# Linear attention ahead of a routed and a dense feed-forward stage: the attention's units put into another order, with smaller tensor tiles for states and turning back

## The reference, cut to what matters

```python
def _attn_ref(q, k, v, alpha):                 # each (4, 8, 768, 48), float32
    state = np.zeros((B, H, D, D)); y = np.zeros_like(q)
    for t in range(S):
        state = alpha[:, :, t, :, None] * state + np.einsum('bhd,bhe->bhde', k[:, :, t], v[:, :, t])
        y[:, :, t] = np.einsum('bhd,bhde->bhe', q[:, :, t], state)
    return y

def reference(...):
    attn_out = _attn_ref(**attn_kwargs)
    x = attn_out.transpose(0, 2, 1, 3).reshape(B * S, H * D)     # 3072 tokens x 384
    x = _moe_ref(x=x, **moe_kwargs)       # normalise, logits against 8 expert vectors, best expert, its relu MLP
    return _moe2_ref(x=x, **moe2_kwargs)  # max of three products with 768 columns, then a product back
```

## Time and profile before

| | us |
|---|---|
| median of 3 runs | 787.59 |
| the runs | 788.26, 786.61, 787.59 |
| the profiled execution | 788.2 |
| its span in the trace | 786.4 |
| end of the attention (last `xc` copied) | 185.86 |

### The profile page before, as it was taken

How to read it: one execution, slowest core, us unless ns; L and a number is a source line. 1 busy time by engine, 2 the same in 40 slices (tenths; PEclk the granted TensorE clock), 3 DMA queues, 4 the chain that set the end, 5 groups by cost and what they waited for, 6 DMA issues and landing times.

```text
span 786.4 us, 15500 instructions
## 1 busy us (share of the span) xinstructions
PE 740.0 (94%) x4774; PEld 652.3 (83%) x4775; DVE 379.5 (48%) x708; ACT 272.5 (35%) x638; POOL 295.8 (38%) x226
## 2 busy tenths in 40 slices
PE   4999999994699999999999999999999999999995
PEld 3888888883499999999999887888888888888885
DVE  6788888865853343333334229433333233333321
ACT  6778888865222222222222231211111112112110
POOL 3243444300382755736358489113133131220011
PEclk9999999997799999999999999999999999999998
DMA  9967675504393443516050220101101010000001
GB/s 181 266 138 180 119 169 106 148 2 144 122 345 128 162 158 133 194 47 218 22 210 31 83 63 21 31 11 40 31 31 51 10 40 30 20 20 0 11 21 50
DMA packets 128790, 74.49 MB, mean 95 GB/s; under 512 B 103448, under 2 KB 122016, under 8 KB 128736
## 3 DMA queue, kind: packets, MB, share of 16 engines
q1 hardware_dynamic: 118624, 53.53, 25.2%
q0 software_dynamic: 4096, 10.24, 3.5%
q10 hardware_dynamic: 6016, 10.07, 3.5%
HBM read 59.03 MB, written 14.79 MB: 94 GB/s over the span
## 4 chain that ended last, share of the span: by engine, by line
PE 77%; issue 13%; DVE 5%; POOL 2%; ACT 1%; DMA 0%; DVEq 0%; POOLq 0%; ACTq 0%
PE bank L1424 54%; PE bank L1223 4%; PE bank L1253 3%; PE bank L1460 3%; PE bank L1316 3%; PE bank L1305 3%; PE bank L1284 2%; PE bank L1297 2%; DVE Sm L893 1%; PE bank L1271 1%; PE bank L1410 1%; POOL out L529 1%; PE bank L1482 1%; DVE A L863 1%; DVE low1h L1044 1%
## 5 line engine op out<-in xcount | busy, mean ns | idle before, releaser
L489 POOL TENSOR_TENSOR wsp<-raw,wsp 128x1536 f32 x28 | 103.8, 3727 | 91.6 <-DVE wsp L1109 91.6
L1424 PE MATMUL bank<-yh,mh 128*128 128x512 f32 x324 | 128.2, 396 | 0.1
L1424 PE MATMUL bank<-yh,ml 128*128 128x512 f32 x324 | 126.5, 390 | 0.0
L529 POOL DMA_INDIRECT out<-oo,tok_t x24 | 24.3, 1011 | 202.5 <-DVE oo L1166 202.5
L1424 PE MATMUL bank<-yl,mh 128*128 128x512 f32 x324 | 91.4, 390 | 0.0
L1424 PE MATMUL bank<-wsp,xh 128*128 (+1 forms) x324 | 85.3, 398 | 3.7 <-issue 3.2
L1424 PE MATMUL bank<-wsp,hTh 128*128 x432 | 81.8, 340 | 0.0
L811 ACT CAST gh<-t 128x512 fp32r<-128x512 f32 x36 | 22.3, 620 | 155.3 <-DVE t L1177 155.3
L1424 PEld LDWEIGHTS bank<-wsp,hTh 128*128 128x128 f32 x432 | 73.9, 188 | 0.2 <-issue 0.2
L1424 PEld LDWEIGHTS bank<-wsp,xh 128*128 128x128 f32 x324 | 58.9, 188 | 15.9 <-issue 4.1
L1424 PEld LDWEIGHTS bank<-yl,mh 128*128 128x128 f32 x324 | 60.8, 188 | 12.9
(11 more groups left out here) (207 smaller groups left out, 1315.4 us busy)
## 6 DMA issues: line engine op xcount, KB each, us to landing
raw<-in_moe_w SPq DMA_DIRECT2D x16, 1536.0 KB, 8.0
expert_rows<-ye ACTq DMA_DIRECT2D x27, 193.0 KB
yg<-expert_rows SPq DMA_DIRECT2D x24, 193.0 KB
nat<-in_alpha SPq DMA_DIRECT2D x32, 144.0 KB, 2.9
nat<-in_k SPq DMA_DIRECT2D x32, 144.0 KB, 3.0
nat<-in_q SPq DMA_DIRECT2D x32, 144.0 KB, 3.0
vt<-in_v SPq DMA_DIRECT2D x32, 144.0 KB, 3.1
attention_rows<-xc SPq DMA_DIRECT2D x4, 1152.0 KB, 5.5
```

The costliest lines, as they stand in the source:

```text
L489: g.tensor_tensor(wsp[:, ds(to, 1), 1, n, part], raw[:, n:n + 1, part], wsp[:, ds(to, 1), 0, n, part].bitcast(f32), ALU.subtract).then_inc ...
L529: g.indirect_dma_start(out=out, out_offset=bass.IndirectOffsetOnAxis(ap=tok_t[:, i, 0:1], axis=0), in_=oo[i % 2][:], in_offset=None).then_ ...
L1424: last = mm(o, x, y, start=(n == 0), stop=(n == len(todo) - 1))
```

## The change

PE's order within a unit becomes: turn `kp`, all scores together, states, results, turn the results of unit u-1 back, carries, turn alpha of u+4, turn q of u+1, turn k of u+2.

- The scores of a unit go to four banks of PSUM (chunks 0 to 3 to banks 6 and 7, chunks 4 and 5 to banks 0 and 1), and DVE masks them with three instructions of 512 elements over two banks each, where it had four of 384.
- States are made per head in tiles of 64 columns: ten products of 48 columns in place of five of 96. `UA` and `V` become 48 wide.
- Turning back is done in four quadrants of 64 by 64: 24 products with N = 56 in place of six with N = 104. It takes the results of the unit before, and those of the last unit are turned back behind the loop. The logits come in eight parts to a token instead of four, so that the reductions at L949 read twice as much. `stage_x` and `store_x` run one unit later.
- DVE's order within a unit becomes three masks, states, scans of u+3, q of u+1, inverse and k of u+2.
- Alpha of unit u+4 is turned (and so needed) at the end of unit u; it was u+3. Alpha, k and q of u+4 are loaded once q of u is turned, v once the results of u are made.
- The first loads stand in the order in which they are needed; two small loads and one alpha are issued by ACT. The norm of the expert vectors is taken with squares on DVE and Ln and Exp on ACT, pads of two buffer sets are written by POOL, and the loops over batches are written out.
- The flag's product moves from the middle of the last unit to its very start.

The core of the diff; `step` is DVE's, and from `back` on it is PE's:

```diff
+        for u in range(NU - UPB):
+            j = u % UPB
+            sp.wait_ge(pe_q, 2 * u + 2)
+            for n in range(3):
+                load_one(u + UPB, j, n)
+            sp.wait_ge(pe_Y, CR + 2 * u + 2)
+            load_one(u + UPB, j, 3)
+            if u and j == 0:
+                store_x(u // UPB - 1)
...
+        def step(u):
+            j = u % UPB
+            for part in range(3):
+                mask(u, j, part)
+            states(u, j)
+            if u + 3 < NU:
+                scans(u + 3, (j + 3) % UPB)
+            if u + 1 < NU:
+                scale_q(u + 1, (j + 1) % UPB)
+            if u + 2 < NU:
+                recip(u + 2, (j + 2) % UPB)
+                scale_k(u + 2, (j + 2) % UPB)
...
+        def back(y, j, b0, c):
+            for half in range(2):
+                rows = slice(HL * half, HL * half + HL)
+                for hd in range(2):
+                    sl = slice(HL * hd, HL * hd + HL)
+                    yield mm(bank[b0 + hd][rows, (D + E) * c:(D + E) * c + D + E], y[sl, c, rows], read[sl, j, :],
+                             start=True, stop=True)
...
             for c in range(CH - 1):
-                last = mm(bank[4 + c // 4][:, HD * (c % 4):HD * (c % 4) + HD].rearrange("p (h d) -> p h d", h=2),
-                          kpT[:, c, :], vt[j][:, c, :, 0:D], start=True, stop=True)
+                for hd in range(2):
+                    rows = slice(HL * hd, HL * hd + HL)
+                    last = mm(bank[4][rows, D * c:D * c + D], kpT[:, c, rows], vt[j][:, c, hd, 0:D],
+                              start=True, stop=True)
             last.then_inc(pe_U, 1)
-            scores(u, j, 1)
...
+            if u:
+                turn_back(u - 1, (j - 1) % UPB)
             for cc in range(1, CH):
...
+            if u + 4 < NU:
+                turn_alpha(u + 4, j, 4)
+            if u + 1 < NU:
+                turn_q(u + 1, (j + 1) % UPB)
+            if u + 2 < NU:
+                turn_k(u + 2, (j + 2) % UPB)
```

More of the change, by code:

```diff
@@ L75, in build @@
     embp = sb("embp", [E, H * HL])
-    read = sb("read", [P, UPB, HD + E])
+    read = sb("read", [P, UPB, D + E])
     es = sb("es", [E, 8])
@@ L217, in build @@
     assert max(attention_end, router_end, experts_end) <= router_const
-    bank = [nc.alloc_psum_tensor(f"bank{i}", [P, 512], f32) for i in range(8)]
+    pair = [nc.alloc_psum_tensor(f"bank{2 * i}_{2 * i + 1}", [P, 2, 512], f32) for i in range(4)]
+    bank = [pair[i // 2][:, i % 2, :] for i in range(8)]
     sem = {}
@@ L329, in _ @@
                          ).then_inc(w0_in, 16)
[L330 to L335, removed]
+        for u in range(NU - UPB):
[7 more added lines that the diff above has]
+                store_x(u // UPB - 1)
+        store_x(B - 2)
         store_x(B - 1)
@@ L429, in _ @@
         pool.sem_inc(const_ready, 1)
+        for j in range(2, NAT):
+            g.memset(nat[j][:, 0, :, :, D:HL], 1.0)
+            g.memset(nat[j][:, 1:3, :, :, D:HL], 0.0)
+            g.memset(vt[j][:, :, :, D:HL], 0.0).then_inc(late_pads, 1)
         def decay(u, j):
@@ L847, in _ @@
             d.memset(vt[j][:, :, :, D:HL], 0.0).then_inc(pads_ready, 1)
+        dve.wait_ge(emb_in, 16)
+        link(d.tensor_tensor(sq[0:E, :], embn[:], embn[:], ALU.mult))
+        d.tensor_reduce(es[:, 0:1], sq[0:E, :], AX.X, ALU.add).then_inc(e_sq, 1)
+        link(d.memset(embp[:], 0.0))
+        dve.wait_ge(ident_ready, 1)
+        for jj in range(UPB):
+            d.tensor_tensor(read[:, jj, 0:D], ident[:, 0:D], ident[:, HL:HL + D], ALU.add)
         dve.wait_ge(e_act, 1)
@@ L1214, in _, with keep_warm @@
         mm, tr = nc.tensor.matmul, nc.tensor.transpose
+        def keep_warm(n, to):
+            for _ in range(n):
+                mm(to[:, 0:HC * P], before[:], causal[:].rearrange("p c n -> p (c n)"), start=True, stop=True)
         pe.wait_ge(ident_ready, 1)
-        pe.wait_ge(pads_ready, NAT)
+        pe.wait_ge(pads_ready, 2)
         def turn(u, j, n, h, dst, done):
@@ L1272, in unit, with scores @@
                 last.then_inc(pe_kT, 1)
+        def scores(u, j):
             pe.wait_ge(dve_qp, CR + 2 * u + 2)
-            pe.wait_ge(act_X, CR + 2 * u)
-            scores(u, j, 0)
-            pe.wait_ge(act_kT, CR + 2 * u + 2)
-            if flag:
+            pe.wait_ge(act_X, CR + 2 * (u - 2) + 2)
+            r = [slice(0, D), slice(HL, HL + D)]
+            for c in range(CH):
+                to = pair[3][:, :, P * c:P * c + P] if c < 4 else pair[0][:, :, P * (c - 4):P * (c - 4) + P]
+                cc = slice(P * c, P * c + P)
+                for hd in range(2):
+                    last = mm(to[:, hd, :], kp[j % 2][r[hd], cc], qp[j % 2][r[hd], cc], start=True, stop=True)
+                    if c in (3, CH - 1):
+                        last.then_inc(pe_S, 1)
@@ L1300, in unit @@
+            for cc in range(CH):
+                if cc % 2 == 0:
+                    pe.wait_ge(dve_S, CR + 3 * u + cc // 2 + 1)
+                for hd in range(2):
+                    mm(out(cc)[HL * hd:HL * hd + HL], vt[j][:, cc, hd, :], Sm[j % 2][:, hd, cc, :],
+                       start=(cc % HC == 0), stop=(cc == 0), skip_group_check=True)
+            if u:
+                turn_back(u - 1, (j - 1) % UPB)
             for cc in range(1, CH):
                 pe.wait_ge(act_UA, CR + 5 * u + cc)
-                pe.sem_inc(pe_carry, 1)
@@ L1380, in _ @@
                     pe.wait_ge(s_yTc, u + 1)
+                    pe.sem_inc(pe_carry, 1)
                     for c in range(CH):
-                        o = (HD + E) * (c % HC)
-                        last = mm(bank[2 + c // HC][:, o:o + HD + E], yT[0][:, c, :], read[:, j, :], start=True, stop=True)
+                        for last in back(yT[0], j, 2, c):
+                            pass
                     last.then_inc(s_X, 1)
@@ L1397, in _ @@
         last.then_inc(r_ss, 1)
-        def keep_warm(n):
-            for _ in range(n):
-                mm(bank[3][:, 0:HC * P], before[:], causal[:].rearrange("p c n -> p (c n)"), start=True, stop=True)
         def lift_x(slot, need, par):
```

288 lines of the change are left out of this document (130 added, 158 removed).

## The result

The changed kernel is faster, by less than half of what was forecast: 781.58 us (median of 8 runs, 777.36 to 784.60) against 786.48 for the kernel before (8 runs, 784.81 to 788.26). The ratio is 0.9931, 95% interval 0.9904 to 0.9958. When it was run a second time, beside the first experiments, it took 779.08 (6 runs) and 0.9912 (0.9890 to 0.9934). Its runs lie 7.2 us apart, those of before 3.5. The profiled execution took 779.84, its span is 778.1 where that of before was 786.4.

A forecast was written before the change was run, and what follows sets the result against it. PE was taken to bound the attention, busy 10.05 of 10.35 us a unit. Units, start, restart, stores, end and last reduction gave 788.2 - 20.7 + 5.4 + 2.4 + 1.0 - 2.5 + 0.4 = 774.2, own range 769 to 779.

The forecast's parts named there:

- -14.0: Whole kernel: the forecast terms' sum in us against the profiled execution of the kernel before, 788.2 to 774.2.
- the end: From unit 12's start to the last copy: 36.5 us instead of 39.0, -2.5, with a 3.6 us wait for the flag.
- the stores: Batch store and alpha load in SP's queue: 8.4 us against 7.7 available, in two units; +1.0, bounds 0 and 2.
- the units: PE's stages per attention unit: 8.47 us instead of 10.35, 1.88 saved in each of 11 units; -20.7.
- behind the last copy: After the attention's last copy: the last reduction, reading twice as much, doubles in time; +0.4 us.
- the start: Until unit 1 begins: +5.4 us waiting for unit 4's alpha, +2.4 for PE's slow restart; together +7.8.
- Quadrants at half rate: Turning back on PE: only two tiles run at a time, 0.61 us more in each of 15 units; 783, chance 0.14.
- small tiles that gain nothing: States and turning back on PE: a slot stays 0.109 us whatever is loaded and moved; 790, chance 0.06.
- one tile at a time: Turning back on PE: quadrants sharing rows or columns wait for each other, 2.0 us more per unit; 804, chance 0.09.
- ACT and DVE did not become the bound: Rival for the attention units: ACT or DVE sets the period, 0.4 to 0.6 us more per unit; 780 to 783, chance 0.10.
- the standstill: End of unit 0: PE idles until unit 4's alpha, queued behind expert 0's large loads, lands at 36.0; +5.4 us.
- a rival without the standstill: End of unit 0: queues serve unit 4's alpha beside the big loads, landing at 29.5; 766 to 767, chance 0.07.

The follow-up runs named there:

- the first experiments: Three single-edit runs against the changed kernel on the same chip: store behind alpha's load, alpha loaded ahead of weights, also POOL's splits later; 776.28, 776.46, 775.24 us.
- the run with the late flag: Changed kernel with the flag's reductions on DVE and product on PE moved behind the last unit's step; 772.20 us, ratio 0.9812.
- the one with pieces: Changed kernel with four edits: unit 4's alpha loaded earlier, expert 0's weights in seven pieces with later splits, stores behind alpha's load, flag behind last unit; 757.71 us.
- the run that filled the wait: Changed kernel with five unused products in PE's wait for the flag ahead of unit 15, the wait itself kept; 777.17 us, ratio 0.9869.
- the run with sixteen products: Changed kernel with sixteen unused products in PE's idle time at the end of unit 0; 777.86 us, ratio 0.9873.
- the run with the store behind: Changed kernel with each batch's store issued behind the load of alpha that it stood ahead of; 776.28 us, ratio 0.9873.
- the run with splits later: Changed kernel with alpha, k and q of unit 4 loaded ahead of expert 0's weights and POOL's splits of them two units later; 775.24 us, ratio 0.9859.
- the run with alpha first: Changed kernel with alpha, k and q of unit 4 loaded ahead of expert 0's two large loads, nothing else; 776.46 us, ratio 0.9869.

## Why the prediction was wrong

**The direction and the mechanisms held, the size didn't.** PE's shorter tiles carry the gain. Of the 5.7 us between -14.0 and -8.3, 2.0 are in the end, 1.75 in the stores, 1.6 in the units and 0.5 behind the last copy; the start gave back 0.2. Quadrants at half rate, small tiles that gain nothing and one tile at a time are ruled out by 0.74 a unit for turning back and 0.69 for the states. The rule of the Trainium skill ("TensorEngine Tiling (Array Packing)", section Instruction Overhead), by which 48 passes were an estimated 1.2 us, does not hold for passes in four quadrants: 0.74 is 15 ns a pass. ACT and DVE did not become the bound of the unit as a whole: its window from 93.77 to 102.39 shows PE busy 8.62 of 8.62, ACT 8.21, DVE 8.18. DVE was put at 7.7 with scans of 2.0; the scans of that unit took 2.67. This cost nothing, since PE was never idle; what DVE did cost are the masks, below.

**The start** was forecast at +7.8 and came at +7.6, with the load's landing (36.46 against 36.0), the standstill and the slow transposes as they were put. The prediction took the lower level from the prologue's transposes of 0.22; the trace of before has no record of the clock ahead of 23.2, and a window there prints 1.00, so that row doesn't show it. The changed kernel's 0.216 at a granted clock of 0.50 does. Against a start with no standstill at all this term is larger than 7.6: taking it away is most of the 14.5 us between the run with the late flag and the one with pieces (2.8 of them are the stores). The forecast had a rival without the standstill at 766; the queue's order settled it the other way.

**The step that failed most by its place in the sum is the end.** It was put at -2.5 and came at -0.5. "Then PE stands at the flag ... that is 3.6 with nothing of PE beside it" was right, 3.41, but "Unit 15 itself is 6.45" counts no clock behind it, though the same prediction counted one behind the standstill. Unit 15 took from its start to turning back 5.93 in the profiled execution and 4.62 in the run that filled the wait (165.68 to 170.30): 1.3 more. In the second traced execution of the changed kernel it was 7.11 (164.47 to 171.58), 2.5 more, and in the run with sixteen products 7.51 (166.40 to 173.91), 2.9 more. So the loss differs from execution to execution. Units 12 to 14 are the rest: with the wait they took 27.30 instead of 26.23, by 0.42, 0.21 and 0.44. With the wait filled the runs lie within 1.2 us and by the lowest of the changed kernel's; I take it that its slower runs lose more there, and that the late flag is worth 6.9 to 9.4 by medians for that reason. It is not shown: the wait and the loss that the traces have come to 4.7 to 6.3, and no execution of the changed kernel above 780 was traced. What is on record of all 14 is the mean granted clock: 0.964 to 0.969 in the seven above 780, 0.968 to 0.974 in the seven below. The Trainium skill ("TensorE: Matmul & The Clock Gate", Part 1) says that the number of products at the low level at a kernel's start differs from run to run of one kernel. Scores of 2.19 and 2.50 behind the flag in two executions of the changed kernel agree with that, inside a kernel.

**The stores** were mis-sized: +1.0 was "0.5 or more, in two units", and it is 2.75, as the run with the store behind shows. The sum took the load as due 7.7 us into the unit. But q and k are turned behind alpha, 1.3 us, which it left out: in unit 5 (start at 74.98) PE was ready for alpha at 81.6, 6.6 into the unit. The store was issued at 75.32, and alpha was there by 83.1.

**The units** were mis-sized by 0.16: 8.63 instead of 8.47. Of the parts, scores (1.54) and transposes (2.76) are exact, turning back and carries 1.94 instead of 2.03. States and results take 2.38 where 2.05 and a wait of 0.08 were forecast, since three masks, 0.60 apart, pace the results. "The last mask covers two chunks only and I leave 0.08" is the failed term: the second and the third mask both hold the results up, not the last alone.

**The base** was 788.2, an execution above the median, and that alone is 0.6 to 1.7 us.

What stays open: whether the clock behind the flag makes up all of the 7 us over which the changed kernel's runs lie, since the traces show losses of 1.3 to 2.9 there. The lower mean clock of the slower runs does not say in which stage it fell.

## What to carry to other kernels

Look at what stands ahead of a small urgent load in its queue, and cut large loads that nobody needs yet into pieces behind the urgent ones: here unit 1 began 12.9 us earlier for it, where all the shorter units together had brought 19. A wait that is harmless by its length can cost the tensor engine's clock for the stage behind it, by an amount that differs from execution to execution; put late checks where nothing follows, or fill the wait. When a consumer is cut into pieces, compare each piece with its producer's time, not only the last one.

## What the runs showed that was not expected

Products in quadrants of 64 by 64 run four at a time: 48 float32 passes in 0.74 us. A change of tile shape costs on both sides: the same 12 passes of turning back take 1.32 between equal shapes and 1.51 between others. And two waits of nearly the same length at the same place of the kernel ended differently: behind 2.71 us (the run with splits later) the granted clock was 1.00 and 18 transposes took 2.02, behind 2.80 (the run with alpha first) it was 0.54 and they took 3.68.
